# Token numbers in the result rows and the squared gate on the finished rows, in a fused attention and expert kernel

## The reference

```python
# 1: attention, 2 batches x 8 heads, 768 positions of 64, masked by cluster
q_assign, k_assign = argmax(q_n @ c_n), argmax(k_n @ c_n)      # 16 centroids a head
attn = softmax(where(q_assign == k_assign, q @ k.T / 8, -1e9))
x = (attn @ v).transpose(0, 2, 1, 3).reshape(1536, 512)
# 2: 8 experts, one for each token
expert_idx = argmax(x @ w_gate)                                  # gate_w: its probability
for e in range(8):
    out[mask] = gate_w[mask, None] * (maximum(x[mask] @ w1[e], 0) @ w2[e])   # 512 -> 1024 -> 512
# 3: a gated layer, 512 -> 1536 -> 512
x = ((x @ w_a) * (x @ w_b)) @ w_out
```

## Time and profile before

| | |
|---|---|
| median of 3 runs | 842.66 us (842.44 to 846.68) |
| the profiled execution | 846.94 us, span 845.2 us |
| granted clock, mean of the span | 0.981 |
| PE busy | 816.7 us, 97% of the span |
| PEld busy | 685.8 us, 81% |
| DVE busy | 459.2 us, 54% |
| POOL busy | 360.6 us, 43% |
| ACT busy | 352.8 us, 42% |
| the chain that ended last | PE 88%, DVE 7%, issue 2% |

### The profile page before, as it was taken

How to read it: one execution, slowest core, us unless ns; L and a number is a source line. 1 busy time by engine, 2 the same in 40 slices (tenths; PEclk the granted TensorE clock), 3 DMA queues, 4 the chain that set the end, 5 groups by cost and what they waited for, 6 DMA issues and landing times.

```text
span 845.2 us, 13127 instructions
## 1 busy us (share of the span) xinstructions
PE 816.7 (97%) x4387; PEld 685.8 (81%) x4388; DVE 459.2 (54%) x736; ACT 352.8 (42%) x711; POOL 360.6 (43%) x297
## 2 busy tenths in 40 slices
PE   7999999999999996999999999999999999999995
PEld 4898898898898584888888888888888888888884
DVE  2779879879887699997778400651211112111110
ACT  1578678678686141343333543212222122121111
POOL 6988988988984261553455554100001000010001
PEclk9699999999999997999999999999999999999998
DMA  7434534544324175776677611410101000010001
GB/s 185 120 93 132 144 97 134 136 105 129 95 78 124 32 248 173 261 242 211 197 245 236 187 38 50 132 44 1 38 13 50 1 12 13 1 50 0 1 1 50
DMA packets 50136, 86.67 MB, mean 103 GB/s; under 512 B 19312, under 2 KB 21360, under 8 KB 50096
## 3 DMA queue, kind: packets, MB, share of 16 engines
q1 hardware_dynamic: 43920, 69.88, 28.2%
q0 software_dynamic: 3440, 11.27, 4.3%
q10 hardware_dynamic: 2736, 4.98, 1.6%
HBM read 73.27 MB, written 11.27 MB: 100 GB/s over the span
## 4 chain that ended last, share of the span: by engine, by line
PE 88%; DVE 7%; issue 2%; POOL 1%; DMA 1%; ACT 0%; SPq 0%; DVEq 0%; POOLq 0%
PE bank L1314 12%; PE bank L1315 12%; PE bank L1316 12%; PE bank L1413 7%; PE bank L1342 7%; PE bank L1217 7%; PE bank L1201 4%; PE bank L1233 4%; PE bank L1207 4%; PE bank L1417 4%; PE bank L1347 4%; PE bank L1235 3%; PE bank L1181 2%; DVE w_split L376 2%; PE bank L1246 2%; PE bank L1354 2%
## 5 line engine op out<-in xcount | busy, mean ns | idle before, releaser
L1148 DVE TENSOR_TENSOR ab_raw<-bank,a_sb 128x512 f32<-128x512 f32 x36 | 24.9, 691 | 191.2 <-PE bank L1316 191.2
L977 DVE TENSOR_REDUCE neg_max<-bank 128x1 f32<-128x768 f32 x96 | 91.7, 955 | 41.0 <-PE bank L1207 40.3
L372 DVE CAST w_split<-stage 128x1024 fp32r<-128x1024 f32 x72 | 65.9, 915 | 76.4 <-PE bank L1347 53.1
L734 ACT ACTIVATE pT_hi<-bank 128x384 fp32r<-128x384 f32 x192 | 85.2, 491 | 49.5 <-PE bank L1217 47.3
L376 DVE TENSOR_TENSOR w_split<-stage,w_split 128x1024 fp32r<-128x1024 f32 x72 | 102.9, 1429 | 2.5
L948 DVE TENSOR_TENSOR pT_lo<-bank,pT_hi 128x384 fp32r<-128x384 f32 x192 | 97.8, 550 | 5.4 <-ACT pT_hi L734 5.2
L755 ACT ACTIVATE probs<-bank,neg_max 128x768 f32<-128x768 f32 x96 | 87.2, 909 | 12.8 <-DVE neg_max L977 12.8
L650 POOL TENSOR_TENSOR hT_lo<-hT_raw,hT_hi 128x512 fp32r<-128x512 f32 x38 | 52.5, 1383 | 92.1 <-ACT hT_raw L793 91.9
L1342 PE MATMUL bank<-w_split,xT_hi 128*128 (+1 forms) x304 | 79.2, 403 | 7.2 <-DVE w_split L376 7.1
L1217 PE MATMUL bank<-ident,probs 128*128 128x128 f32 x576 | 83.0, 279 | 1.2 <-DVE pT_lo L948 1.1
L1413 PE MATMUL bank<-w_split,hT_hi 128*128 (+1 forms) x304 | 79.5, 403 | 0.5 <-issue 0.5
(11 more groups left out here) (223 smaller groups left out, 1719.4 us busy)
## 6 DMA issues: line engine op xcount, KB each, us to landing
stage<-w SPq DMA_DIRECT2D x64, 512.0 KB, 4.3
q_raw<-qT SPq DMA_DIRECT2D x32, 192.0 KB, 3.7
k_raw<-kT SPq DMA_DIRECT2D x32, 192.0 KB, 3.9
sorted_y<-y_sb ACTq DMA_DIRECT2D x19, 256.0 KB, 3.9
q_pair<-qT SPq DMA_DIRECT2D x8, 384.0 KB, 4.6
k_pair<-kT SPq DMA_DIRECT2D x8, 384.0 KB, 4.9
v_raw<-v_keys SPq DMA_DIRECT2D x16, 192.0 KB, 4.2
stage<-w_a SPq DMA_DIRECT2D x6, 512.0 KB, 4.2
```

The costliest lines, as they stand in the source:

```text
L977: dve.tensor_reduce(neg_max[:, qt % 2:qt % 2 + 1], scores[qt % 2][:, 0:S], AX_X, ALU.max, negate=True).then_inc(s_max, 1)
```

## The change

1. **The token columns.** A row of `sorted_y` has two more numbers, the token's row in the output and its row in a gate table. DVE makes them for all slots from the slot lists, and ACT writes them with one DMA into columns 512 and 513. When rows are gathered for layer two, the numbers come along; POOL saves them as integers (`save_rows`). No lists of tokens or gates by place are made.
2. **The places** follow from counts: place plus the padding of all experts before it (`find_places` on DVE, ten small instructions behind expert 2's chunks). `make_place_one_hots`, PE's `find_places` and the seven instructions behind it go.
3. **The gate.** DVE squares it, ahead of the slot lists; ACT writes it to DRAM (`gate_rows`), POOL gathers it in twelve DMAs in layer two, and `copy_out` scales the finished rows. `scale_rows` goes.
4. **One-hot matrices** for the first tile are made by two wide instructions instead of twelve, those for all slots by one.
5. **The first four high parts of expert 1** are made by ACT when attention's last product is done; DVE makes their low parts alone.
6. **PE's order.** 21 spins instead of 19; the slot product comes directly behind the first transposes, with one spin instead of three behind it.
7. ACT's loop over tiles is written out; POOL makes two more constants.

```diff
         def make_high(eng, i, dst):
...
+            if i < HELD:
                 eng.tensor_tensor(dst[:, 0], src, factors[:, 1:2].to_broadcast([P, CH]), ALU.mult).then_inc(s_cvp, 1)
+            elif i < HELD + C1:
+                eng.activation(dst[:, 0], src, ACT.Copy).then_inc(s_cva, 1)
             else:
                 eng.tensor_copy(dst[:, 0], src).then_inc(s_cvh, 1)
...
             def gather_y(t):
                 y_tiles = Y_TILES[t // 4]
                 if t >= 2:
                     pool.wait_ge(s_TX2, t - 1)
+                    save_rows(t - 2)
+                    pool.wait_ge(s_tk, t - 1)
...
+            def save_rows(t):
+                pool.wait_ge(s_yg[t % 2], (t // 2 + 1) * 16)
+                pool.tensor_copy(token2_i[:, t], x2[:, t % 2, DM:ROW]).then_inc(s_tk, 1)
+            def gather_gates(g):
+                pool.wait_ge(s_tk, 4 * g + 4)
+                for t in range(4 * g, 4 * g + 4):
+                    pool.indirect_dma_start(out=gate2[:, t:t + 1], out_offset=None, in_=gate_rows, ...
...
+            def first_high(c):
+                make_high(act, HELD + c, w_split[:, chunk_at(1, c)])
+            act.wait_ge(s_back, 2 * G)
+            first_high(0)
+            first_high(1)
             act.wait_ge(s_gx, 1)
             act.activation(l_exp[:, :, :], l_dif[:, :, :], ACT.Exp).then_inc(s_ge, 1)
+            first_high(2)
+            first_high(3)
+            act.wait_ge(s_gate, 1)
+            act.dma_start(gate_rows.rearrange("(p t) o -> p (t o)", p=P), gate[:, :]).then_inc(s_grow, 16)
...
             relu(0, 0)
+            act.wait_ge(s_trd, 1)
+            act.dma_start(sorted_y[:, DM:ROW].rearrange("(j p) o -> p j o", p=P), token_row[:, :, :]).then_inc(s_trow, 16)
             relu(0, 1)
...
-                act.activation(out_buffer(t), out_ps[t % 4], ACT.Copy).then_inc(s_o, 1)
+                act.wait_ge(s_g2[t // 4], 64)
+                act.activation(out_buffer(t), out_ps[t % 4], ACT.Copy, scale=gate2[:, t:t + 1]).then_inc(s_o, 1)
...
-            for t in range(T):
-                dve.tensor_scalar(lane_hot[:, t, :], row_no[:, 0, :], first_key[:, t:t + 1], -1.0, ...
+            for tiles in (slice(0, T // 2), slice(T // 2, T)):
+                dve.tensor_tensor(lane_hot[:, tiles, :], row_no1[:, :, :].to_broadcast([P, T // 2, P]),
+                                  first_key[:, tiles].unsqueeze(2).to_broadcast([P, T // 2, P]), ALU.is_equal).then_inc(s_fhot, 1)
...
             dve.tensor_tensor(first_i[:, :], first_token[:, 1:2], first_f[:, :], ALU.add).then_inc(s_first, 1)
+            dve.wait_ge(s_ge, 1)
+            link(dve.tensor_reduce(l_sum[:, :], l_exp[:, :, :], AX_X, ALU.add))
+            link(dve.tensor_scalar(l_sum[:, :], l_sum[:, :], 1e-9, None, ALU.add))
+            link(dve.reciprocal(gate[:, :], l_sum[:, :]))
+            dve.tensor_tensor(gate[:, :], gate[:, :], gate[:, :], ALU.mult).then_inc(s_gate, 1)
...
-            for t in range(T):
-                dve.tensor_scalar(row_hot[:, t, :], row_no[:, 0, :], slot_lane[:, t:t + 1], None, ALU.is_equal).then_inc(s_thot, 1)
+            dve.tensor_tensor(row_hot[:, :, :], row_no[:, :, :].to_broadcast([P, T, P]),
+                              slot_row[:, :].unsqueeze(2).to_broadcast([P, T, P]), ALU.is_equal).then_inc(s_thot, 1)
...
+            link(dve.tensor_scalar(token_g[:, :], slot_token[:, 1], float(T), None, ALU.mult))
+            dve.tensor_tensor(token_row[:, :, 0], slot_token[:, 1], token_f[:, :], ALU.add)
+            dve.tensor_tensor(token_row[:, :, 1], slot_token[:, 0], token_g[:, :], ALU.add).then_inc(s_trd, 1)
...
+            def find_places():
+                link(dve.tensor_scalar(pad[:, :], n_tiles[:, :], float(P), None, ALU.mult))
+                link(dve.tensor_tensor(pad[:, :], pad[:, :], counts_f[:, :], ALU.subtract))
...
+                dve.tensor_tensor(back_i[:, :], place_no[:, :, 0], shift[:, :], ALU.add).then_inc(s_place, 1)
...
             def convert(i, dst):
-                make_high(dve, i, dst)
+                if i >= HELD + C1:
+                    make_high(dve, i, dst)
                 make_low(dve, i, dst)
...
-                if r == 1:
-                    make_place_one_hots()
                 if r == 2:
-                    dve.wait_ge(s_placeT, 1)
...
+                    find_places()
...
-            spin(19)
+            spin(21)
...
             transpose_x(0, 0)
-            spin(3)
+            find_slots()
+            spin(1)
             hidden(0, 0, 0, 0)
-            find_slots()
             hidden(0, 0, 1, 0)
```

More of the change, by code:

```diff
@@ L309, in attention_moe_gate @@
         s_yout = [sem(f"y_written{i}") for i in range(2)]
-        s_packed = sem("place_values_packed")
-        s_phot = sem("place_one_hots_done")
-        s_placeT = sem("place_values_in_psum")
         s_place = sem("places_done")
         s_yg = [sem(f"y_gathered{i}") for i in range(2)]
-        s_x2 = sem("x2_scaled")
+        s_gate = sem("gates_done")
+        s_grow = sem("gates_written")
+        s_g2 = [sem(f"squared_gates_landed{i}") for i in range(3)]
+        s_trd = sem("token_columns_done")
+        s_trow = sem("token_column_written")
+        s_tk = sem("output_rows_saved")
         s_TX2 = sem("x2T_in_psum")
@@ L828, in _ @@
             copy_y(0, 0)
-            def tile(j, par):
-                later = not static(j) or j + 1 < TILES
-                if later:
+            for j in range(TILES):
+                par = j % 2
+                if j + 1 < TILES:
                     relu(j + 1, 0)
-                if not static(j) or j >= 1:
+                if j >= 1:
                     store_y(j - 1, 1 - par)
                     hT_out(j, 1)
-                if not static(j) or j + 2 < TILES:
+                if j + 2 < TILES:
                     xT_out(j + 2, par)
-                if later:
+                if j + 1 < TILES:
                     relu(j + 1, 1)
                     hT_out(j + 1, 0)
-                if static(j) and EARLY < j <= EARLY + 4:
+                if EARLY < j <= EARLY + 4:
                     x2T_out(j - EARLY - 1)
-                if not static(j) or j >= 1:
+                if j >= 1:
                     copy_y(j, par)
-                if static(j) and EARLY <= j < EARLY + 4:
-                    scale_rows(j - EARLY)
-            over_tiles(act, tile)
             store_y(TILES - 1, (TILES - 1) % 2)
@@ L1367, in transpose_x2 @@
                 last.then_inc(s_TX2, 1)
-            def find_places():
-                pe.wait_ge(s_phot, 1)
-                for t in range(T):
-                    last = pe.matmul(place_ps, lane_hot[:, t, :], place_values[:, t], start=(t == 0), stop=(t == T - 1))
-                last.then_inc(s_placeT, 1)
             def weight(n, k, f):
@@ L1456, in tile @@
                 expert_out(j, 1, r)
-                if static(j) and j == 1:
-                    find_places()
             over_tiles(pe, tile)
```

132 lines of the change are left out of this document (54 added, 78 removed).

## The result

The changed kernel takes 841.44 us (median of 20 runs, 838.19 to 844.11), the kernel before, run beside it, 843.26 us (20 runs, 842.31 to 848.95): a ratio of 0.996, 95% interval 0.9943 to 0.9978. It is faster, by 0.2 to 0.6%, and not by the 1.3% that was predicted. The predicted range ended at 837.5 us. Its profiled execution took 838.19 us (span 836.4), its fastest; that of before took 846.94. So the two profiles lie 8.75 us apart and the medians 1.8.

What follows compares the result with a forecast made beforehand. TensorE, busy 97%, was held at tile 3 by VectorE's late `w_split` chunks and then ran at low clock. 9.2 + 2.64 - 0.6 - 0.1 = 11.1 us, so 842.66 becomes 831.5, range 829.5 to 837.5.

Steps and rivals of the forecast that it cites:

- The wait and its clock: At tile 3's hidden product: 9.2 us of lateness and 2.64 us of slow clock would go.
- the cover: At tile 3: expert 2's four chunks would be ready 2.8 us or more before TensorE arrives.
- The start of the experts: From attention's end to the experts: slot lists, spins and the low-part conflict would together start them 0.6 us late.
- The price of 0.30 us for a spin: In the routing before the transposes: two more spins would cost 0.4 to 0.6 us, taken as 0.5.
- one VectorE low part in front of `xT_lo`: At POOL's first `xT_lo`: upper bound of 1.2 us on a delay taken as 0.4.
- the low price: Token-column write at about 292: 7 us scaled from 256-byte pieces; 7 to 10 us of landing taken.
- the long price: Token-column write: 25 us scaled from 32-byte pieces; as a rival, loads held up, about 848 us, 4%.
- the twelve output copies get a scale: Layer two: scale from SBUF costs 0 to 0.1 us per copy, only the last on the path: 0.1.
- needed only at the twelfth unit of each group, so 0: Layer two: POOL's twelve small index saves and twelve 512-byte gathers, issued while it waits for TensorE, cost 0.
- The stretch in question: Between attention and layer two: same work in profiled and median runs, so the median also falls by 11.1 us.
- three rivals: Wait shrinks only, 837.1 (15%); token columns hold queue, about 848 (4%); expert 2 waits otherwise, within 2 us of 842.7 (3%).
- signs of being wrong: `w_split` wait at tile 3 or 5, chunk loads 10 us+ after 291, `x_in` wait at 299, first hidden product after 289.5.

Runs made afterwards that it cites:

- j1: The kernel before, unchanged, profiled once more: 842.71 us.
- j4: The changed kernel, unchanged, profiled a further time: 840.32 us.
- j3: The changed kernel, unchanged, profiled once more: 843.58 us.
- f3: Changed kernel with x2 allocated behind x2T_a, plus five wide unread VectorE instructions where the lists were: 847.62 us (1.0024 of before).
- j2: The kernel before, unchanged, profiled a further time: 846.50 us.
- f2: Changed kernel with x2 allocated behind x2T_a and POOL's two new constants made after its first pair of heads: 835.54 us.
- f5: Changed kernel with x2 behind x2T_a, 256 bytes of room ahead of x2T_a, and token columns written at tile 3: 833.74 us, one execution.
- e4: Changed kernel with 32 unused bytes ahead of x2T_a and POOL's two new constants made after its first pair of heads: 838.97 us.
- g1: f2 without the twelve gate gathers, scaling with another token's gate, so output is wrong: 835.45 us (0.9886 of before).
- h1: Changed kernel with x2T_raw and x2 allocated behind x2T_a and the two new constants made later: 834.80 us, one execution.

## Why the prediction was wrong

**The wait and its clock: right.** 9.2 + 2.64 = 11.84 us were forecast. Measured, from the first hidden product to layer two, are 13.0 us between the first profiles and 248.42 - 236.58 = 11.84 between `j1` and `j4`. That the second is the forecast to the last digit is luck: between `j1` and `j3`, which both have slow clock in the routing, it is 248.42 - 237.84 = 10.6. `f3` shows the mechanism from the other side. Tile 3 came at 318.41, 2.6 us before the forecast 321, mostly since the profiled execution was already 2.2 us ahead at the first hidden product (286.59 against 288.8). That the cover was 2.8 us was wrong: it was 0.5 us in this profile, and 2.0 at most in any. Late loads (3.70, 0.47 and 0.58 us of idle time at expert 1's last four chunks) and chunks of up to 2.9 us took the rest. The right outcome had little to spare.

**The start of the experts: two cases where one was forecast.** 0.6 us late were forecast. Like has to be compared with like here, since both the profile of before and `j1` have slow clock in the routing. Without it the routing takes 12.73 us after and 12.68 before (288.40 - 275.72 in `j2`): 0.05 us late. With it, it takes 13.52 us in `j3` against 13.26 in `j1`, 0.3 us late, and another 1.26 us go until layer two (237.84 against 236.58). The price of 0.30 us for a spin mixed the two clocks, since slow clock fell among the 19 spins of the earlier trace rows: at full clock 21 take 4.69 us, 0.22 each. The bound "one VectorE low part in front of `xT_lo`" is that second case: 2.16 us instead of 1.28. By the Trainium skill ("SBUF — State Buffer", Who interferes with whom) such a pair of instructions keeps each other waiting entirely, and the traces agree. In the eight profiles of the changed kernel and its variants in which VectorE came first, POOL's instruction took 2.16 us, 0.88 more. In the seven others POOL came first and took 1.28 to 1.29; in one of them, `f2`, VectorE's low part fell into it and took 1.75 us instead of 1.24. Those eight are the profiles with slow clock in the routing.

**The token columns: the low price was right.** 7 to 10 us of landing were forecast and 7.5 measured (in the profiles that write them at tile 0 it is 7.3 to 9.5, but for one of 12.3 and one of 14.6); by pieces of the 32-byte row it would have been 25 us. For 19 KB that is long, beside 2.3 us for 192 KB in 768 pieces of 256 bytes. Whether the rule of the Trainium skill on transfers under 512 bytes ("DMA: Bandwidth & Descriptors", Specifications), which stood behind the long price, has a part in it, no run here shows; the long price it did not bring. Its neighbours paid: 3 to 4 us of idle VectorE.

**Layer two: this step failed.** I priced it as "the twelve output copies get a scale ... only the last on the path: 0.1" and "needed only at the twelfth unit of each group, so 0" for the gathers. The copy was right (0.69 us instead of 0.60). But two more numbers in each of the two rows of `x2` moved `x2T_a` and cost 4.8 us, and twelve indirect DMAs cost 1.0 us in a drain at the very end, off every path that I had followed. 5.84 us against 0.1. The sum had no term for where a buffer lies, and none for the end of an engine's program.

**From the profile to the median: this step failed too.** "The stretch in question is the same work in both, so the median becomes 842.66 - 11.1." The work is the same and its price is not: the slow clock at tile 3 was worth 1.2 us less in the executions near the median. What the rest is, `j1` and `j4` show, each within 1.2 us of its kernel's median: attention +3.81 us (275.74 - 271.93), routing -0.54 (slow clock in `j1` and none in `j4`, not the change), experts -11.84, layer two and tail +6.07 (313.46 - 307.39), together -2.5 us. Attention's code is the same but for two constants, worth 0.3 us (its last product at 272.19 in `f5`, at 271.9 with the constants later in `e4`, `g1` and `h1`, all four with the same slow stretch at the start), and the kernel before has executions with that product at 275.7 as well. Whether the change makes these more frequent, or the runs drew them, is not settled: in four programs with the constants moved 12 of 24 runs had a mean clock of 0.990 or more, in six with them ahead 16 of 59.

**What the chances said.** None of the three rivals is what happened, and a result within 0.5% of before, as this one is, had been given 4%. Two of the signs of being wrong did come, outside the first profile: in `e4` a chunk load issued at 291.48 lands after 10.6 us, and TensorE waits for `x_in` at 297.81. Neither is where the 5.84 us went. Of smaller things, the places take eight instructions and 2.9 us, not ten and 2.4, and nothing waits for them.

With the address mended and the constants moved the median is 835.5, at the predicted range's upper part (829.5 to 837.5), and 833.8 with the rest; 1.0 us of the distance to 831.5 is the drain.

## What to carry to other kernels

A change that makes any buffer longer moves all that are allocated behind it: compare the mean duration of the commonest matmuls, streamed tensor by streamed tensor, in the profiles before and after. If one group differs by 2% at the same shape, look at the distance between its two operands before any theory of the schedule. Price an edit in the part of the kernel where "nothing waits" too, down to the last instruction of each engine. A gain read from one profiled execution includes that execution's slow clock; profile both kernels more than once before a gain of 1% is put on a median.

## What the runs showed of the hardware that I had not expected

- A matmul of 128x512 with a stationary 128x128 in fp32r is issued every 0.227 us when the tensor of the streamed operand starts 0, 256 or 2048 bytes behind that of the stationary one, modulo 4096, every 0.233 us at 32 bytes and on average every 0.230 us at 64. Moving all tensors by 32 bytes changes nothing.
- GpSimd's DRAIN at the end of the program takes 3.579 us after 43 indirect DMAs and 4.559 us after 55, in every profile taken here (5 and 14 of them; 0.0817 us for each on average).
- A ScalarE copy of 1024 elements from SBUF takes 1.0 us, inside the 0.63 to 1.26 of the prediction.
- Executions of the same kernel differ by 4 us through the slow clock in the first 60 us (842.71 and 846.50 us of before: 6.8 and 20.5 us of it there). A stretch of 3.4 us of it in the routing goes with another order behind it: in the changed kernel and its variants VectorE was ahead of POOL at the first `xT_lo` in all eight profiles with it and in none of the seven without.
